# Mixture-of-experts kernel on one core: another order of work within an expert tile, and weight loads in 512 runs of 4 KB

## What is computed

```python
# layer 1: attention of x (8, 8, 512, 64) against state (8, 8, 32, 64), both ways; 4352 rows of 512 come out
# layer 2: h = x @ w_in (512 x 2048); g = h * clip(h + 3, 0, 6) / 6; x = g @ w_out (2048 x 512)
# layer 3:
logits = x @ w_gate                       # 8 experts
e_idx = np.argmax(logits, axis=1)
for e in range(E):
    mask = e_idx == e
    h = np.maximum(x[mask] @ w1[e], 0.0)  # 512 -> 1024
    ye = h @ w2[e]                        # 1024 -> 512
    out[mask] = gate_w[mask, None] * eom[mask, e, None] * ye
```

## Time and profile before

| | us |
|---|---|
| median of 3 runs (lowest, highest) | 1167.43 (1164.4, 1169.1) |
| the profiled execution, its own time | 1165.16 |
| its span, first to last instruction | 1163.3 |
| TensorE busy in the span | 1121.6 (96%) |
| VectorE, ScalarE busy | 639.1 (55%), 467.1 (40%) |
| granted TensorE clock, mean of the span | 0.985 |

### The profile page before, as it was taken

One profiled execution on the slowest core, in us unless ns is written; L12 is line 12 of the kernel. 1 busy time (PEld: TensorE's weight loads), 2 busy tenths in 40 slices (PEclk: granted clock), 3 DMA queues, 4 the chain that ended last, 5 costly groups with the idle time before them and its releaser, 6 DMA issues.

```text
span 1163.3 us, 20895 instructions
## 1 busy us (share of the span) xinstructions
PE 1121.6 (96%) x6358; PEld 887.2 (76%) x6359; DVE 639.1 (55%) x1247; ACT 467.1 (40%) x780; POOL 77.0 (7%) x96
## 2 busy tenths in 40 slices
PE   9999999999999999999999988989999999979995
PEld 7777777777777777777778977767888888858884
DVE  6675654655646556556564347546474445556632
ACT  4554434443444344434544351425343223344420
POOL 0000100101001001010010110010110010101111
PEclk9999999999999999999999989999999999989998
DMA  9210111102101111020020275667675444847542
GB/s 366 90 37 7 67 37 37 43 32 74 37 6 69 37 37 41 33 74 1 1 110 1 101 245 179 217 237 233 203 248 180 153 145 130 282 149 215 161 139 65
DMA packets 98783, 131.36 MB, mean 113 GB/s; under 512 B 13967, under 2 KB 75023, under 8 KB 94352
## 3 DMA queue, kind: packets, MB, share of 16 engines
q1 hardware_dynamic: 91360, 89.35, 24.3%
q10 hardware_dynamic: 1584, 23.07, 5.5%
q0 software_dynamic: 5760, 17.90, 4.0%
HBM read 85.86 MB, written 45.47 MB: 113 GB/s over the span
## 4 chain that ended last, share of the span: by engine, by line
PE 85%; DVE 4%; DMA 3%; issue 3%; ACTq 2%; ACT 1%; SPq 1%; DVEq 0%; POOL 0%; POOLq 0%
PE y_ps L855 33%; PE h_ps L837 15%; PE y_ps L928 13%; PE y_ps L912 7%; PE h_ps L912 6%; PE a_ps L812 2%; PE h_ps L827 2%; DMA hidden<-expert_hid 1%; DMA hid_mv<-hidden 1%; ACTq L444 1%; DVE we L483 1%; PE a_ps L715 1%; PE a_ps L796 1%; SPq L609 1%; PE a_ps L776 1%
## 5 line engine op out<-in xcount | busy, mean ns | idle before, releaser
L855 PE MATMUL y_ps<-w_out_hi,hid_hi 128*128 128x512 f32 x544 | 217.6, 400 | 0.0
L855 PE MATMUL y_ps<-w_out_hi,hid_lo 128*128 128x512 f32 x544 | 212.2, 390 | 0.0
L855 PE MATMUL y_ps<-w_out_lo,hid_hi 128*128 128x512 f32 x544 | 212.0, 390 | 0.0
L928 PE MATMUL y_ps<-we,act_t_hi 128*128 (+1 forms) x608 | 189.0, 392 | 6.2 <-DVE act_t_lo L1559 3.6
L1365 DVE SCALAR_TENSOR_TENSOR hid<-hid,h_ps 128x512 f32<-128x512 f32 (+1 forms) x144 | 94.5, 656 | 166.3 <-ACT hid L1035 164.7
L837 PE MATMUL h_ps<-att_hi,mix 128*128 128x512 f32 x512 | 184.0, 402 | 0.1
L1035 ACT ACTIVATE hid<-h_ps,three 128x512 f32<-128x512 f32 (+1 forms) x144 | 95.5, 663 | 174.8 <-PE h_ps L837 151.4
L855 PEld LDWEIGHTS y_ps<-w_out_hi,hid_hi 128*128 128x128 f32 x544 | 102.1, 188 | 49.9 <-issue 30.4
L928 PEld LDWEIGHTS y_ps<-we,act_t_hi 128*128 128x128 f32 x608 | 114.6, 189 | 31.9 <-issue 8.2
L1374 DVE TENSOR_TENSOR hid_lo<-hid,hid_hi 128x512 fp32r<-128x512 f32 (+1 forms) x144 | 94.9, 659 | 70.5 <-ACT hid_hi L1043 69.5
L1552 DVE STREAM_TRANSPOSE act_raw<-hid_mv 128x512 f32<-128x512 f32 x76 | 49.5, 690 | 136.2 <-DMA hid_mv<-hidden 134.8
(11 more groups left out here) (216 smaller groups left out, 1409.5 us busy)
## 6 DMA issues: line engine op xcount, KB each, us to landing
raw<-in_w ACTq DMA_DIRECT2D x11, 2048.0 KB, 8.4
hidden<-expert_hid SPq DMA_DIRECT2D x76, 256.0 KB
hid_mv<-hidden SPq DMA_DIRECT2D x152, 128.0 KB
xg<-buckets SPq DMA_DIRECT2D x164, 64.0 KB
xb<-in_x_rows SPq DMA_DIRECT2D x8, 1024.0 KB, 4.9
x_t<-in_x_t SPq DMA_DIRECT2D x7, 1024.0 KB, 4.9
buckets<-pad_row SPq DMA_DIRECT2D x8, 774.0 KB, 8.0
raw<-in_w SPq DMA_DIRECT2D x3, 2048.0 KB, 7.5
```

The costliest lines, as they stand in the source:

```text
L855: i = pe.matmul(y_ps[:, t, :], (hid_hi, hid_lo)[hp][:, hid_at(b, j), t * P:(t + 1) * P], w_out_s[wp][:, j, :], start=(j == 0 and m == 0), ...
L928: i = pe.matmul(y2_ps[:, slot % 2, :], act_t[hp][:, slot % 2, f, :], we[:, bass.ds(w_at + (wp * WPART + KD * F + f * DM), DM)], start=(f = ...
```

## The change

1. ACT's order is now: load_w1 (tile after a marked one), split_hi of w1 (marked tile), relu(t), rows_hi(t+2), hidden_hi(t-1), split_hi of w2, load_w2.
2. DVE's order is now: put_out(t-3), split_lo of w1, turn_rows(t+2), rows_lo(t+2), turn_hidden(t-1), hidden_lo(t-1), split_lo of w2.
3. The rows of tile 1 are turned and split while DVE still computes the table, no longer after it.
4. The marks for splitting and loading are one column (0, 1 or 2) instead of two, which is one small DVE operation and up to two register loads fewer.
5. The weights lie in DRAM piece by piece, so that a load of 2 MB is 512 runs of 4 KB instead of 128 runs of 16 KB.

```diff
-        sp.dma_start(raw1[:], w1[0].rearrange("p k f -> p (k f)")).then_inc(sem("raw1_loaded"), 16)
+        sp.dma_start(by_pieces(raw1), w1[0].rearrange("i p c -> p i c")).then_inc(sem("raw1_loaded"), 16)
...
         split_hi(1, 0, 0)
         rows_hi(Tile(0, 0))
+        rows_hi(Tile(0, 1))
         act.wait_ge(sem("table_ready"), 1)
...
         def body(t):
-            if not t.last:
-                rows_hi(t.plus(1))
-            split1 = entry(act, t, T_SPLIT)
+            split1 = entry(act, t, T_SPLIT, 2)
+            before_it = t.plus(-1)
             if not t.first:
+                split2 = entry(act, before_it, T_SPLIT, 2)
+                with act.If(split2 > 1):
+                    n = entry(act, before_it, T_ORD, E - 1) + 1
+                    load_w1(entry(act, before_it, T_NEXT, E - 1), n + 1)
+            with act.If(split1 > 0):
+                ...
+                wait(act, "hid2_ps", HALVES * t.n)
+                split_hi(0, n, other)
             for h in range(HALVES):
                 ...  # relu
+            if not (isinstance(t.n, int) and t.n + 2 >= MT):
+                rows_hi(t.plus(2))
             if not t.first:
                 hidden_hi(t.plus(-1))
...
                 with act.If(split2 > 0):
                     ...
-                    with act.If(load > 0):
-                        load_w1(e, n + 1)
                     if not is_b(t.n, 1):
                         wait(act, "y2_ps", first_tile)
                     split_hi(1, n, other)
-                    with act.If(load > 0):
-                        load_w2(e, n + 1)
-            with act.If(split1 > 0):
-                ...
-                split_hi(0, n, other)
+                    with act.If(split2 > 1):
+                        load_w2(entry(act, before_it, T_NEXT, E - 1), n + 1)
```

More of the change, by code:

```diff
@@ L196, in sc @@
         return at(name, scratch[0] - -(-n // 32) * 32, shape, dtype)
-    T_ROW, T_LIVE, T_FINAL, T_ORD, T_SPLIT, T_LOAD, T_NEXT, T_SLOT, T_OTHER, T_FIRST, T_N = range(11)
+    T_ROW, T_LIVE, T_FINAL, T_ORD, T_SPLIT, T_NEXT, T_SLOT, T_OTHER, T_FIRST, T_N = range(10)
     MT = MAX_TILES
@@ L227, in emit_kernel @@
     upto_n = at("upto_n", st_diag_at + 1344, [P, E, E], F32)
-    passed = at("passed", sread_at + 2048, [P, MT, E], F32)
+    passed = at("passed", 147456, [P, MT, E], F32)
     assert MT * E * 4 <= 1344 and E * E * 4 <= 704 and MT * E * 4 <= 2048
@@ L1490, in _ @@
         rows_lo(Tile(0, 0))
+        turn_rows(Tile(0, 1))
         chain(dve.tensor_scalar(slot_n[:], slot_back[:], total[:], None, ALU.add))
@@ L1503, in _ @@
         chain(dve.tensor_copy(table[:, T_ORD, 0:MT], t_ord[:]))
+        rows_lo(Tile(0, 1))
         chain(dve.tensor_tensor(t_chg[:, 0:MT - 1], t_ord[:, 1:MT], t_ord[:, 0:MT - 1], ALU.subtract))
@@ L1512, in _ @@
                                        op0=ALU.is_lt, op1=ALU.mult))
-        chain(dve.tensor_copy(table[:, T_SPLIT, 0:MT], t_start[:]))
-        chain(dve.scalar_tensor_tensor(out=t_start[:], in0=t_left[:], scalar=-2.0, in1=t_chg[:],
+        chain(dve.scalar_tensor_tensor(out=t_chg[:], in0=t_left[:], scalar=-2.0, in1=t_chg[:],
                                        op0=ALU.is_lt, op1=ALU.mult))
-        chain(dve.tensor_copy(table[:, T_LOAD, 0:MT], t_start[:]))
+        chain(dve.tensor_tensor(table[:, T_SPLIT, 0:MT], t_start[:], t_chg[:], ALU.add))
         chain(dve.tensor_scalar(t_next[:], t_ord[:], 3.0, None, ALU.add))
@@ L1528, in _ @@
         dve.sem_inc(sem("table_ready"), 1)
-        turn_rows(Tile(0, 1))
         def put_out(t):
@@ L1563, in body @@
         def body(t):
-            if not t.last:
-                rows_lo(t.plus(1))
+            if not (isinstance(t.n, int) and t.n < 3):
+                put_out(t.plus(-3))
+            split1 = entry(dve, t, T_SPLIT, 2)
+            if not t.first:
+                split2 = entry(dve, t.plus(-1), T_SPLIT, 2)
             if t.first:
                 split_lo(dve, 1, 0, 0, range(1, PIECES), "w2_ready")
[L1568 to L1573, removed]
+            with dve.If(split1 > 0):
+                split_lo(dve, 0, entry(dve, t, T_ORD, E - 1) + 1, entry(dve, t, T_OTHER, WSLOT), signal="w1_ready")
             if not (isinstance(t.n, int) and t.n + 2 >= MT):
                 turn_rows(t.plus(2))
+                rows_lo(t.plus(2))
             if not t.first:
+                turn_hidden(t.plus(-1))
                 hidden_lo(t.plus(-1))
```

29 lines of the change are left out of this document (13 added, 16 removed).

## The result

The changed kernel takes 1173.05 us (median of 18 runs, 1163.81 to 1177.62), the kernel before, run in turns with it, 1165.75 (18 runs, 1161.52 to 1171.98). The ratio is 1.0053 with a 95% interval of 1.0036 to 1.0071: slower by about 6 us, where 1147 was forecast. The profiled execution took 1172.2, its span is 1170.5. Two executions of later kernels, of 3951.98 us (`loadearly16`) and 3132.36 us (`turnfirst4k`), are left out of the ratios.

What follows compares the result with a forecast made beforehand. TensorE was taken to bound the kernel. Gains of 6.95, 11.61 and 4.10 (22.7 us) less losses of 0.9, 0.2 and 1.2 (2.3) gave 20.4 net, a median of 1147 us; own range 1143 to 1151.

Steps and rivals of the forecast that it cites:

- the part on the load of w1: Earlier load in 4 KB runs: stores beside it take 6.0 instead of 9.52 us, nothing counted for `hid_mv`; gain 4.10.
- The 5.4: Room in us for the hidden values in an undisturbed tile, with the rows ahead of their transposes; later delays draw on it.
- slower than before: Rival: early load_w1 holds back marked tile's `hid_mv` and the next store; 4.7 us at each of five changes, 1179; chance 0.06.
- First weights' split at the head: Tile 28's first block: the wait for its weights' split and the slow clock go, gain 11.61 us.
- Rows two ahead: Rows made two tiles early: three waits for `xg_t_lo`, at first blocks of tiles 4, 5 and 9, go; gain 6.95 us.
- Second(4), 4.10: Second block of tile 4: its 2.40 us wait for hidden values and 1.70 of slow clock go; lower bound nothing.
- the rival of bursts: Load's turns are 8 to 16 runs of 4 KB, so stores wait nearly as long as with 16 KB: 1150; chance 0.09.
- turns run by run: DMA engines alternate single runs between load and store, so 4 KB shortens a store beside a load by 3.5 us; 1147.
- runs do nothing: Rival: runs of 4 KB have no effect, tile 3's store takes 9.5 us, its second block is 4.0 late; 1153 to 1159; chance 0.08.
- New waits, 1.2: Later second blocks, mainly tiles 28 and 29 at about 0.9 late each: 0 to 4 us lost, 1.2 taken.
- Start: Table ends at 714.1, first matmul block starts near 715.2: 0.2 us lost, bounds 1 gained and 1.5 lost.
- Tail, 0: Last block's wait for its hidden values: SP's order is untouched, so no change, 0 us.

Runs made afterwards that it cites:

- loadearly16: Kernel before with only load_w1 moved ahead of relu in the tile after a marked one, runs of 16 KB: 1181.37 us, ratio 1.0125.
- turnfirst4k: Changed kernel with the hidden values' transposes ahead of the rows of tile t+2 on DVE, and hidden_hi ahead of rows_hi on ACT: 1175.07 us, ratio 1.0067.
- w1late16: Changed kernel with load_w1 back behind hidden_hi, ahead of the second weights' split, and weights in runs of 16 KB: 1151.56 us, ratio 0.9896 to the kernel before.
- w1late4k: Changed kernel with load_w1 back behind hidden_hi, ahead of the second weights' split, runs of 4 KB kept: 1153.06 us, ratio 0.9900 to the kernel before.
- splitonly16: Kernel before with only the first weights' split moved to the head of the marked tile, runs of 16 KB: 1154.57 us, ratio 0.9901.
- order16: Changed kernel with the old weight layout, runs of 16 KB: 1169.61 us, ratio 1.0043 to the kernel before.
- before4k: Kernel before, in its old order, with the new weight layout, runs of 4 KB: 1167.28 us, ratio 1.0020.

## Why the prediction was wrong

**The step that failed** is in the part on the load of w1: "For `hid_mv`, 64 rows of 512 B an engine, more than 32 runs either way, I count nothing." The moved load was priced only for the stores behind it. Issued ahead of relu(t+1), it starts in tiles 2 and 6 while the `hid_mv` of the marked tile t are being issued (741.29 and 742.24 above), and takes that of tile 2 from 2.88 to 10.82. That is 7.9 late. The four blocks of room held 3.7 of it (in `w1late16` the transposes start at 743.91, values are ready 2.94 later by the changed kernel's 754.08 and 757.02, and second(2) is due at 739.70 + 10.88 = 750.6), and 4.62 became a wait, with the slow clock behind it. At second(12) the same omission works through the tile behind: for such a tile the prediction had a store of 6.0 and a `hid_mv` of 5.5, and they took 8.74 and 9.40.

The room was wrong too. The 5.4 was counted for an undisturbed tile. In a marked tile relu comes about 5 later, behind the split (734.30 for 728.98 in tile 2), as the prediction says in its own paragraph on the price, and it did not take that off. By its own figures 21.8 (second(2) is due) less 10.8 (the transposes start), 5.3 (relu's delay) and 3.3 (the copies) is 2.4, to which second(1)'s own wait of 1.57 adds.

In all the load's place is worth 17 to 18 us, 3.5 for each of five loads, but very unevenly. The waits at second(2), (3), (6), (7) and (12) are 14.2 of the 19.8, and 0.3 of them is left in `w1late4k`. The change in tile 24 cost no wait, that in tile 27 at most the 1.09 at second(28).

**The rival that came true** is the last but one, "slower than before", by its mechanism: both the `hid_mv` of the marked tile and the store behind it are held back, though not at each of the five changes. I gave it 0.06. Its price of 4.7 a change was too high as a mean, and the gain to be beaten too: 12 in place of 20.4. The error lay in what spoke against it: "in 812 to 1018 two changes passed without any wait". In the kernel before, load_w1 stood behind hidden_hi(t), which needs the landed `hid_mv` of t, so the marked tile's own transfer could not meet it there. But the trace of before does hold this pair one tile later, at one of those two calm changes, and I didn't look at it (timeline of the kernel before):

```profile
855.17 2.57 SPq L609 DMA_DIRECT2D hid_mv<-hidden  x4
...
856.54 0.35 ACTq L1119 DMA_DIRECT2D raw<-in_w  x1
...
866.33 1.30 DVE L1552 STREAM_TRANSPOSE act_raw<-hid_mv 128x512 f32<-128x512 f32 x2 [0.41 <-DMA hid_mv<-hidden]
```

The transposes of tile 12 start 8.6 after the last issue has ended (857.74). One tile on, with no load beside it, they start 2.3 after (876.09, 878.38). So the transfer was 6.3 late there as well, and second(12), at 871.40, did not wait, since it needs the transposes only 3.3 earlier. The calm showed room in the old order, not a free transfer. Against the 3.7 of room that tile 2 has in the new one, 6.3 late is a wait of 2.6 and the slow clock behind it, above the 2.4 from which the rival decides. The 7.47 of the earlier trace rows says the same more weakly (4.6 late). I had instead taken 5.5 for an undisturbed transfer, from half of a chain of 10.8, which hid most of the difference. What sets the time of such a transfer between 6.4 and 10.9 was not settled.

Term by term:

- **First weights' split at the head**: right. Forecast 11.61 less 0.9 at second(1), 10.7; alone it measured 11.5 (0.99%). In the changed kernel TensorE has no wait for `we` (1.58 at first(28) in `w1late16`), and the clock at 1018 to 1040 is 1.00. second(1) waits 1.78 (forecast 2.8).
- **Rows two ahead**: the waits went as forecast, but no gain of 6.95 shows. Over the split alone it is 0.05% (0.9901 to 0.9896), with intervals that leave 4 us open either way, and 3.7 in the lost time of one execution each (20.4 to 16.7). Without the split at the head it is a loss. A likely reason, not shown by a run of its own: the waits for rows had pushed the following second blocks back, so that the hidden values were in time there; without them the values are what is late. How the new waits divide between this and the rows' steps on ACT and DVE was not settled.
- **Second(4), 4.10**: the wait and its slow clock did go, for a reason that isn't the one given. It is gone in the changed kernel and in `w1late16`, with 4 KB and with 16 KB alike, and 0.45 in `w1late4k`; `splitonly16`, with 16 KB, has 0.65. So it left with the order. The term rested on stores of 6.0 beside a load, and none was that short. The store of tile 4 behind load_w2 takes 7.51 and 8.68 (chain of `w1late4k`) with 4 KB, and 7.07 (`order16`), 7.66 (`w1late16`) and 9.52 with 16 KB:

```profile
761.85 8.68 DMA hidden<-expert_hid
```

  The 9.52 was the long end of a spread, not the price of runs of 16 KB. By the Trainium skill ("DMA: Bandwidth & Descriptors", "Queues, rings and completion order") an engine takes whole packets of several descriptors from a queue before it turns to the next. By that rule the rival of bursts follows, stores nearly as long as with 16 KB, and on this point the 7.51 and 8.68 side with it against my turns run by run. They fit "runs do nothing" as well, and prove no rule.
- **New waits, 1.2**: waits for `act_t_lo` are 19.8 in 9, against 6.8 in 6 in `w1late4k`, with the same runs and the load late. So about 13 of them come from the failed step.
- **Start**: right. The table ends at 714.05 (forecast 714.1), first(1) starts at 715.97 (715.2).
- **Tail, 0**: the last block waits 2.72 (2.48 before), but takes 7.36 for 5.75, at a granted clock of 0.77. In `before4k`, whose order is the old one, it takes 7.36 too, so it doesn't take the new order; the cause stays open.

From the forecast gain of 20.4 to the measured loss of 6.2 are 26.6. By the ratios about 17.2 of them are the load's place (`w1late16` to `order16`), 1.2 the runs of 4 KB (`order16` to the changed kernel, within the noise), and 8.3 what the rest of the order gave less than forecast: 12.1 (1.04%) for 20.4. Of these 8.3 the trace of `w1late16` shows 3.8 lost at second(5), second(7) and second(29), for which 1.2 had been counted, and 1.9 at first(28), for which nothing had. The others can't be told from the spread between executions.

## What to carry to other kernels

Before a transfer is issued earlier, ask which transfers its old place had let land first: an order can act as a guard, and then a stretch of the old trace without waits says nothing of the collision. Look for the same pair elsewhere in that trace, where it has room and so costs nothing, and read its price there. Then take the room of the very tile that is hit, less what the same change has already taken from it; or let the large transfer wait for the landing of the small one. And count a removed wait as gain only after looking at what would be late next behind it.

## What was unexpected of the hardware

- A group of four DMAs of 128 KB (`hid_mv`, small rows) takes 2.7 to 4.0 in the chains where no weight load runs beside it, and mostly 7.4 to 10.9 beside a load of 2 MB from another queue (6.38 once, where the load came with the last of the four, and 14.81 beside two loads), whether the load comes in runs of 4 KB (10.82, 9.90) or of 16 KB. In the chain of `order16`:

```profile
743.14 9.84 DMA hid_mv<-hidden
...
794.04 10.85 DMA hid_mv<-hidden
```

- The load pays too: its median landing went from 8.0 to 10.2 in the changed kernel (7.5/10.2/11.5), where the runs of 4 KB alone add 0.5 in the old order (`before4k`) and the order alone 1.0 (`order16`, 9.0).
- Taking 2 MB loads out of five places of a loop was worth 2.1%, though TensorE never waited for a load itself.
